# A three-stage kernel: routed rows loaded in blocks and turned by VectorE instead of TensorE, register reads split, a table built inside a branch

## What is computed

```python
x = attention(q, k, v).transpose(0, 2, 1, 3).reshape(3072, 512)
logits = x @ w_gate                      # 8 experts
expert_idx = argmax(logits, axis=1)
for e in range(8):
    mask = expert_idx == e
    out[mask] = gate_w[mask, None] * (np.maximum(x[mask] @ w1[e], 0) @ w2[e])   # 512 -> 1024 -> 512
h = out @ w_in                           # 512 -> 2048
g = (a0 + a1*h + a2*h**2 + a3*h**3) / (1 + |b0|*|h| + |b1|*h**2 + 1e-6)
return g @ w_out                         # 2048 -> 512
```

## Time and profile before

| what | value |
|---|---|
| median of three runs | 1125.18 us |
| the profiled execution | 1128.27 us, its span 1126.7 us |
| mean granted TensorE clock | 0.993 |
| TensorE busy | 1095.6 us, 97% |
| VectorE busy | 898.5 us, 80% |
| ScalarE / GpSimd busy | 593.5 / 259.6 us |
| attention | 0 to about 212 us |
| hand-over to the experts | 212 to 241 us |
| expert tiles | 241 to 585 us |
| dense stage | 585 to 1127 us |

### The profile page before, as it was taken

The page is one execution under the profiler, slowest core; times in us unless marked ns, Lnnn a source line. Parts: engine busy times, 40 slices in busy tenths (PEclk is TensorE's granted clock), DMA queues, the critical chain, the costliest instruction groups (busy, mean ns, idle before and its releaser), DMA issues.

```text
span 1126.7 us, 19523 instructions
## 1 busy us (share of the span) xinstructions
PE 1095.6 (97%) x6023; PEld 891.4 (79%) x6024; DVE 898.5 (80%) x1813; ACT 593.5 (53%) x1060; POOL 259.6 (23%) x191
## 2 busy tenths in 40 slices
PE   6999999799999999999999999999999999999997
PEld 4777777578888888888887888888888888888885
DVE  6778888658788887878769988987986986996975
ACT  6878788322323232322338656655665655655663
POOL 1022111364656566563500001001001001000101
PEclk9999999999999999999999999999999999999999
DMA  8999871296767877875621010010001001000000
GB/s 195 242 281 266 194 200 40 89 327 197 271 220 259 289 240 251 291 242 193 248 94 49 1 39 38 1 38 37 0 1 74 0 0 66 9 0 10 29 1 38
DMA packets 142362, 142.52 MB, mean 126 GB/s; under 512 B 104672, under 2 KB 104672, under 8 KB 141280
## 3 DMA queue, kind: packets, MB, share of 16 engines
q0 software_dynamic: 27584, 92.48, 23.6%
q1 hardware_dynamic: 114720, 49.31, 16.3%
HBM read 118.70 MB, written 23.32 MB: 126 GB/s over the span
## 4 chain that ended last, share of the span: by engine, by line
PE 88%; DVE 8%; ACT 1%; issue 1%; DMA 1%; POOL 0%; SPq 0%; POOLq 0%; ACTq 0%; DVEq 0%
PE bank L1145 23%; PE bank L1147 23%; PE bank L1146 23%; PE bank L990 4%; PE bank L966 4%; PE bank L953 4%; PE bank L931 2%; PE bank L1140 1%; PE bank L1006 1%; DVE poly L1749 1%; DVE poly L1747 1%; PE bank L1215 1%; DVE poly L1762 1%; PE bank L1015 1%; DVE bank L1635 1%
## 5 line engine op out<-in xcount | busy, mean ns | idle before, releaser
L1635 DVE STREAM_TRANSPOSE bank<-hbuf 32x256 f32<-32x256 f32 x464 | 211.5, 456 | 62.0 <-ACT hbuf L766 55.5
L488 POOL TENSOR_TENSOR w_lo<-stage,w_hi 128x2048 fp32r<-128x2048 f32 x32 | 147.6, 4613 | 60.1 <-DMA w_hi<-in_moe_w_dram 28.9
L1145 PE MATMUL bank<-w_hi,gh 128*128 128x512 f32 x384 | 150.5, 392 | 0.3 <-DVE gl L1771 0.3
L1145 PE MATMUL bank<-x2Th,w_hi 128*128 128x512 f32 x384 | 149.5, 389 | 0.5 <-DVE poly L1749 0.5
L1147 PE MATMUL bank<-w_hi,gl 128*128 128x512 f32 x384 | 149.5, 389 | 0.0
L1146 PE MATMUL bank<-w_lo,gh 128*128 128x512 f32 x384 | 149.4, 389 | 0.0
L1147 PE MATMUL bank<-x2Th,w_lo 128*128 128x512 f32 x384 | 149.4, 389 | 0.0
L1146 PE MATMUL bank<-x2Tl,w_hi 128*128 128x512 f32 x384 | 149.4, 389 | 0.0
L623 POOL DMA_INDIRECT out_dram<-stage,ids x24 | 29.6, 1235 | 510.1 <-ACT stage L875 494.4
L1145 PE MATMUL bank<-w_hi,xTh 128*128 (+1 forms) x248 | 97.9, 395 | 2.2 <-DVE xTl L1623 1.5
L1147 PE MATMUL bank<-w_hi,xTl 128*128 (+1 forms) x248 | 97.6, 393 | 0.0
(11 more groups left out here) (221 smaller groups left out, 2221.1 us busy)
## 6 DMA issues: line engine op xcount, KB each, us to landing
w_hi<-in_moe_w_dram POOLq DMA_DIRECT2D x32, 1024.0 KB, 7.6
stage<-in_moe_w_dram POOLq DMA_DIRECT2D x32, 1024.0 KB, 8.0
xg<-routed_x SPq DMA_DIRECT2D x31, 256.0 KB, 4.8
routed_y<-ybuf SPq DMA_DIRECT2D x31, 256.0 KB, 2.7
x<-routed_y SPq DMA_DIRECT2D x6, 1056.0 KB, 5.1
kraw<-in_k_dram SPq DMA_DIRECT2D x24, 256.0 KB
qraw<-in_q_dram SPq DMA_DIRECT2D x24, 256.0 KB
vraw<-in_v_dram SPq DMA_DIRECT2D x24, 256.0 KB, 4.8
```

Source lines behind the costliest of these rows:

```text
L488: pool.tensor_tensor(w_lo[:, at:at + CH], stage[:, c % 2, :], w_hi[:, at:at + CH].bitcast(F32), ALU.subtract).then_inc(chunk_ready, 1)
L1145: pe.matmul(dst, lhs_hi, rhs_hi, start=first, stop=False)
L1635: ins = dve.transpose(HB_ps[k][r * QD:(r + 1) * QD, :, q % 2 * QD:(q % 2 + 1) * QD], rows)
```

## The change

Rows are written to `routed_x` with their columns in another order: `turn_x` writes each transpose in four quarters, so that a row holds its 512 values as [4][4][32]; `normalise`, `normalise_last`, `invert` and `weigh_logits` follow that order, with the reciprocals kept twice. A tile is then loaded by four DMAs of 32 partitions each (512-byte pieces), and one VectorE operation of 128x512, made of 32x32 blocks, gives what TensorE's four transposes gave. VectorE does it (`turn_rows`) ahead of `turn_h` of the tile before; its loop now holds two tiles. The first x tile's four DMAs are issued two by SyncE and two by ScalarE. TensorE reads two registers ahead of `moe_down` and two ahead of `moe_up`. The whole table is built inside each side of the `If`, all 26 linked steps ahead of the first tile; the second tile is turned right behind the first, into a bank and buffers of its own, so TensorE's first tiles run as up(0), first half of up(1), turn of h(0), second half of up(1). The unread products are spread: 7 while the last pair is picked, 16 behind the count, one for each of the steps 16 to 26, four when x(0) is turned. GpSimd's first fetch waits for both first tiles.

```diff
             def load_x(t, r, first=False):
...
-                sp.dma_start(xg[:, r, :], xs[ds(row, P), 0:DM]).then_inc(xg_in[r], 16)
+                load_rows(r, row)
+            def load_rows(r, row, parts=range(4)):
+                for a in parts:
+                    sp.dma_start(xg[a * QD:(a + 1) * QD, r, :].rearrange("n (b c) -> n b c", b=4),
+                                 xs[ds(row, P), a * P:(a + 1) * P].rearrange("(b n) c -> n b c", b=4)).then_inc(xg_in[r], 16)
...
-            sp.dma_start(xg[:, 0, :], xs[0:P, 0:DM]).then_inc(xg_in[0], 16)
+            load_rows(0, 0, (0, 1))
...
-            pool.wait_ge(xg_in[0], 16)
+            pool.wait_ge(xg_in[0], 64)
+            pool.wait_ge(xg_in[1], 64)
...
-            moe_x(0)
-            moe_h(0); moe_x(1); end_ht(0, hTh)
+            for p in range(QT // 2):
+                act.wait_ge(routed[p], 32 * B)
+            for a in (2, 3):
+                act.dma_start(xg[a * QD:(a + 1) * QD, 0, :].rearrange("n (b c) -> n b c", b=4),
+                              xs[0:P, a * P:(a + 1) * P].rearrange("(b n) c -> n b c", b=4)).then_inc(xg_in[0], 16)
+            moe_x(0); moe_x(1, XS_ps, xSh)
+            moe_h(0); end_ht(0, hTh)
...
             def turn_x(b, i, full=False, n=None):
...
-                    mm = pe.transpose(dst[:, j * P:(j + 1) * P], oT[:, i % 2, j, :], ident[:, :])
+                    mm = pe.transpose(quarters(dst[:, :], j), oT[:, i % 2, j, :], ident[:, :])
...
+            def idle_while_picking():
+                pe.wait_ge(chunk_ready, 1)
+                pe.wait_ge(lg_read, LAST + 1)
+                idle_products(1)
+                pe.wait_ge(lg_sum, LAST + 1)
+                idle_products(1)
+                for step in range(4):
+                    pe.wait_ge(lg_step, 4 * (LAST // 2) + step + 1)
+                    idle_products(1)
+                pe.wait_ge(oh_step, LAST // 2 + 1)
+                idle_products(1)
...
-                idle_products(WARM[0])
+                idle_products(WARM)
...
-            idle_products(WARM[1])
+            pe.wait_ge(chunk_ready, 1)
+            for step in range(16, TAB_STEPS + 1):
+                pe.wait_ge(tab_step, step)
+                idle_products(1)
...
-            def pe_tile(t, r, n):
-                off_down, e_down, off_up, e = weights_at(t - 1), expert_of(t - 1), weights_at(t + 1), expert_of(t + 1)
-                moe_turn_x(r, n)
+            def pe_tile(t):
+                off_down, e_down = weights_at(t - 1), expert_of(t - 1)
                 moe_down(t - 1, off_down, e_down)
+                off_up, e = weights_at(t + 1), expert_of(t + 1)
                 moe_up(t + 1, off_up, e)
...
-            moe_turn_x(0, 1)
-            moe_up(0, 0, 0)
+            pe.wait_ge(xg_ps, 1)
+            idle_products(4)
+            moe_up(0, 0, 0, halves=(0,))
             pe.wait_ge(tab_ready, 1)
             off, e = weights_at(1), expert_of(1)
-            moe_turn_x(1, 1)
+            moe_up(0, 0, 0, halves=(1,))
+            moe_up(1, off, e, xSh, xSl, (0,))
             turn_end_h(0)
-            moe_up(1, off, e)
-            pe_tile(1, 0, 2)
+            moe_up(1, off, e, xSh, xSl, (1,))
+            pe_tile(1)
...
-                dve.reciprocal(rcp[:, i % 2, 1, :], rcp[:, i % 2, 0, :]).then_inc(rc_step, 1)
+                dve.reciprocal(rcp[:, i % 2, :, :, :],
+                               den[:, i % 2, :].rearrange("p (j u o) -> p u o j", u=2, o=1).broadcast_to([P, 2, 2, KB]))\
...
+            def turn_rows(t, r, n, dst=X_ps):
+                dve.wait_ge(xg_in[r], 64 * n)
+                if dst is X_ps and not (isinstance(t, int) and t == 0):
+                    dve.wait_ge(xg_lo, t)
+                dve.transpose(dst[:, :].rearrange("p (j b n) -> p j b n", j=KB, b=4),
+                              xg[:, r, :].rearrange("p (b j n) -> p j b n", j=KB, b=4)).then_inc(xg_ps, 1)
...
             with dve.If(banded(dve) > 0):
                 dve_steps()
+                expert_tables()
...
-            def dve_tile(t):
-                turn_h(t, 0); moe_x(t + 1); turn_h(t, 1); moe_ht(t)
-            moe_x(1); end_ht(0, hTh, hTl)
-            with dve.Fori(1, MT - 2) as t:
-                dve_tile(t)
+            def dve_tile(t, r, n):
+                turn_rows(t + 1, r, n); turn_h(t, 0); moe_x(t + 1); turn_h(t, 1); moe_ht(t)
+            end_ht(0, hTh, hTl)
+            with dve.Fori(0, (MT - 3) // 2) as tp:
+                for r in range(2):
+                    dve_tile(2 * tp + r + 1, r, tp + 2)
+            turn_rows(MT - 1, 0, MT // 2 + 1)
```

More of the change, by code:

```diff
@@ L41 @@
 TI = 13
-WARM = (18, 8)
+WARM = 16
+TAB_STEPS = 26
 FAR = -8e9
@@ L139, in build_program @@
         sums = over("sums", [P, 2, H])
-        rcp = over("rcp", [P, 2, 2, H])
+        den = over("den", [P, 2, H])
+        rcp = over("rcp", [P, 2, 2, 2, KB])
         zeros = over("zeros", [P, RW])
@@ L163, in build_program @@
         early = free[1]
+        x2_at = free[1]
         x2 = over("x2", [P, G, RW])
+        xSh, x2_at = place("xSh", [P, KB, P], F32R, x2_at)
+        xSl, _ = place("xSl", [P, KB, P], F32R, x2_at)
         x2Th = over("x2Th", [P, KB, G * P], F32R)
@@ L194, in build_program @@
         HT_ps = bank[2:4]
+        XS_ps = bank[6]
         HB_ps = [bank[2 + k].rearrange("p (j n) -> p j n", j=FB) for k in range(2)]
@@ L694, in evac_logits, with head_cols @@
                 act.activation(lgT[:, :], X_ps[:, 0:P], ACT.Copy).then_inc(lt_sb, 1)
+            def head_cols(row, h):
+                return row.rearrange("p (u v j n) -> p u v j n", u=2, v=2, j=KB)[:, h % 2, :, h // 2, :]
             def normalise_last():
@@ L992, in weigh, with quarters @@
                 mm.then_inc(pv_done, 1)
+            def quarters(row, j):
+                return row.rearrange("p (a j n) -> p a j n", a=4, j=KB)[:, :, j, :]
             def turn_x(b, i, full=False, n=None):
@@ L1032, in route_rank, with idle_products @@
                     .then_inc(rank_ps, 1)
+            def idle_products(times):
+                for n in range(times):
+                    pe.matmul(HT_ps[1][:, :], w_hi[:, 0:P], w_hi[:, 0:512], start=True, stop=True)
+            def idle_while_picking():
[9 more added lines that the diff above has]
+                idle_products(1)
             def pe_steps():
@@ L1108, in count @@
                 pe.matmul(X_ps[:, 0:E], ones[:, :], taken[:, NT // 2 % 2, 0, :], start=True, stop=True).then_inc(count_ps, 1)
[L1110 to L1114, removed]
             with pe.If(banded(pe) > 0):
@@ L1134, in expert_of @@
                 return pe.value_load(exp_i[0:1, 0, ds(t, 1)], min_val=0, max_val=E - 1)
[L1136 to L1141, removed]
             def three(dst, lhs_hi, lhs_lo, rhs_hi, rhs_lo, first, last):
@@ L1147, in three, with moe_up @@
                 return pe.matmul(dst, lhs_lo, rhs_hi, start=False, stop=last)
-            def moe_up(t, off, e):
+            def moe_up(t, off, e, hi=xTh, lo=xTl, halves=(0, 1)):
                 pe.wait_ge(chunk_ready, e * 4 + 2)
                 pe.wait_ge(xg_lo, t + 1)
-                for n in range(2):
+                for n in halves:
                     if not isinstance(t, int) or t > 0:
@@ L1586, in _ @@
                         low_part(b, n)
[L1588 to L1612, removed]
@@ L1613, in _ @@
-            for k in range(2):
-                tl(dve.tensor_tensor(prod[:, k, :, :], past, per_expert(wide[:, 0, k, :]), ALU.mult))
-            tl(dve.tensor_reduce(ttab[:, 0:2, :], prod[:, 0:2, :, :], AX.X, ALU.add))
-            tl(dve.tensor_tensor(ttab[:, 0, :], ttab[:, 0, :], row_no[:, :], ALU.add))
-            tl(dve.scalar_tensor_tensor(out=ttab[:, 2, :], in0=ttab[:, 1, :], scalar=last_at[:, 0:1], in1=ttab[:, 0, :],
-                                        op0=ALU.add, op1=ALU.min))
@@ L1619, in _ @@
-            dve.tensor_copy(row_i[:, :], ttab[:, 2, :]).then_inc(row_ready, 1)
-            def moe_x(t):
-                dve.wait_ge(xg_hi, t + 1)
-                dve.tensor_tensor(xTl[:, :, :], X_ps[:, :].rearrange("p (j n) -> p j n", j=KB), xTh[:, :, :].bitcast(F32),
-                                  ALU.subtract).then_inc(xg_lo, 1)
+                expert_tables()
             def turn_h(t, k):
```

93 lines of the change are left out of this document (64 added, 29 removed).

## The result

The median is 1116.42 us (four runs, 1114.92 to 1118.07); the kernel before took 1125.6 on the same chip (1124.7 to 1126.33). The ratio is 0.9917 with an interval of [0.9904, 0.993]: 9.2 us gained where 15.1 were predicted. The sign is right, but the time lies 0.9 us above the range. The profiled execution took 1118.07 us, span 1116.4, against a span of 1126.7 before: 10.3 us less.

A forecast was written before the change was run, and what follows sets the result against it. TensorE, busy 97% of the span, was taken to bound the kernel. Transposes 11.9, hand-over order 1.8 and clock 1.4 sum to 15.1 us off the median of 1125.18: 1110.1 us, range 1106.1 to 1115.5.

The forecast's parts named there:

- 1. Transposes leave TensorE: Expert tiles: without x transposes on TensorE, 27 tiles give back 0.44 us each, 11.9 us; bounds 2.2 us either way.
- 2. VectorE's new operation: VectorE's gap before turning h: the block transpose takes 0.72 us, fits in 1.34 us idle, and costs nothing.
- The last tile: End of the expert tiles: TensorE waits there for VectorE's scaling, so what this tile saves is waited away.
- 3. Loading in four parts: Loads of x tiles: four DMAs instead of one cost nothing; the longest landing, at most 15.4 us, still fits.
- 4. Reads in two places: TensorE's register reads, two ahead of down and two ahead of up: cost nothing; bounds 0 and 0.2 us a tile.
- 5. The tables: Hand-over: tables inside the `If` start near 212.4, end about 221.2; up(0) stays at 224.66, bounds -0.3 and +0.9 us.
- 6. The order in the hand-over: up(0) to down(0) shrinks from 16.46 to 11.8 us at full clock; counted 1.8 plus 1.4, the middle of 0 to 2.85.
- (c): TensorE exposes waits the transposes covered, at reads or for `hTl`: 0.2 us a tile, 5.4 less gain, 1115.5 us; 9%.
- (a): VectorE sets the pace because the block transpose runs by quadrants, 3.66 us: slower, about 1175 us; 3%.
- (b): The back edge of VectorE's two-tile loop stalls 2.91 us each two tiles: slower, 1133 us; 3%.
- (d): Hand-over: the tables aren't earlier, as the 2.91 us idle aren't the jump: gain 11.8, 1113.4 us; 9%.
- (e): Whole kernel: no difference, some hold-up takes all of the gain; 2%.

The follow-up runs named there:

- e7: Changed kernel, but VectorE turns each tile's rows twice, the second time into a bank nobody reads: 1113.42 us, ratio 0.9915 to the kernel before.
- e1: Changed kernel, but the next tile's `xTl` is made after four of the first eight block transposes of h: 1110.69 us, ratio 0.986 to the kernel before.
- e3: Changed kernel, but VectorE turns the last x tile behind `gate_shift(0)` instead of ahead of it: 1115.13 us, ratio 0.9904 to the kernel before.
- e6: Changed kernel, but SyncE issues all four DMAs of the first x tile, ScalarE none: 1115.17 us, ratio 0.9894 to the kernel before.
- e2: Changed kernel, but TensorE's four register reads of a tile stand together ahead of down: 1122.23 us, ratio 0.9966 to the kernel before.
- e4: Changed kernel, but tables and the first two tiles' turns stand once behind the `If`: 1118.1 us, ratio 0.9922 to the kernel before.
- e0: Changed kernel measured again without any edit: 1115.48 us, ratio 0.9907 to the kernel before.

## Why the prediction was wrong, point by point

**1. Transposes leave TensorE: the mechanism right, the gain not all there.** 11.9 us were predicted, 8.8 - 1.2 = 7.6 came. With `xTl` early the 28 tiles give 319.12 - 304.64 = 14.5 us, more than 28 x 0.44 = 12.3. The pace without transposes is 0.2267 us a product and not the 0.2278 that I read out of the earlier trace rows, so 10.88 a tile and not 10.93: the sets disturbed later products too, which stood in the prediction as a bound of +2.2. Another 0.6 us are two tiles of 11.72 and 11.65 in the trace of before, where the others take 11.37 or 11.38.

**2. VectorE's new operation: the price right, its cover wrong. This is the step that failed.** 0.72 was predicted, 0.727 measured. I looked for its cover in the gap ahead of the h turn, found 1.34 us, and then looked at only one result behind it, `hTl` (0.5 in hand). I put the cost of this step at nothing. But the new operation is not what took the time: e7 doubles it and loses nothing. The lost time is of the other result in the same chain: ReLU of the second half, eight block transposes, `xTl`, up. That chain hangs on the *previous up*, so it doesn't move when down starts sooner; up does, by the 0.44 that the transposes took. Of the 0.64 in hand 0.16 were left, and TensorE starts its product 0.23 behind the end of `xTl` (so in 28 tiles of after, the last among them, and 0.20 behind in the first). With the late second product that is 0.18 us a tile, and 0.20 was lost (11.08 for 10.88). What the change saved it took from a slack that I had not read. Undoing the lateness alone (e1) brings 5.7 us back in the 28 tiles, more than the 3.5 that were missing there.

The Trainium skill ("VectorE: DVE Perf Modes", Rules for kernel authors), which would have left the transposes on TensorE, agrees with the durations here (0.727 us on VectorE; the four transposes cost a tile of TensorE's 11.37 - 10.88 = 0.49). It doesn't fit this kernel, where TensorE sets the pace and VectorE has idle time.

**The last tile** was to lose what it saved (0.4 by the table above) and lost 1.2. The scaling was named, but not that `turn_rows(30)` was put ahead of `gate_shift(0)`, with ScalarE's exp and ReLU behind it. e3 gives 0.7 of it back.

**3. Loading in four parts: right.** In the loop nothing waits for it (VectorE waits 2.2 us for x(0) and x(1), in the hand-over); the longest landing, 11.6 us, lies within the bound of 15.4. In e6 ScalarE's part doesn't show.

**4. Reads in two places: the number right, the reason wrong.** "Nothing" holds for two and two (e1). But the four reads in one place showed no gap before, with transposes behind them, and without these they cost 6.7 us (e2). That the transposes hid them is the likely reading; no run has them back with the reads as they are. Without the split more than half of the gain would be gone (3.8 of 10.5 us left), and I had priced it as a side matter.

**5. The tables: right.** 212.78 for "near 212.4", ready at 221.56 for 221.2, and e4 shows the jump. Where the jump now falls VectorE has 7.06 us to wait for ScalarE's `hTh` in any case (229.11 to 236.17). up(0) at 225.46 instead of 224.66 (bounds -0.3 and +0.9) goes with the first load, which the scatter let go at 220.29 instead of 219.31.

**6. The order in the hand-over: right in its order, the clock open.** At full clock (e0) up(0) to down(0) takes 236.03 - 224.16 = 11.87 us; 11.8 was predicted. In after, with the clock at half for its first products, it is 13.07. So the end of the term with all 2.85 kept occurs, and the end with nothing doesn't: in after 1.2 us are lost, not 2.85. Of the thirteen traces of the changed kernel and its variants ten show 11.9 us and three 13.0 to 13.1. The middle value was low, and luck had a part in it. What decides between the two is open.

**The rivals.** *(c)* was near in price (0.2 us a tile, 1115.5) but named the reads and `hTl`; it was `xTl`. At 9% I held it too unlikely, for the one slack I had read spoke against it. It also set the high end of the range, 1115.5, with every other term at its middle, which left no room for the 0.8 us more that the last tile lost. *(a)* and *(b)* fall: VectorE has 0.73 us idle a tile, and no back edge of its loop shows (its tiles take 11.07 to 11.10 us by turns). *(d)* and *(e)* fall with e4 and the median.

**The sum again**: 7.6 + 2.6 + 0.1 = 10.3 us of span. The gain of the medians is 9.2, since the profiled execution before was 2.7 us above its median and that of after 1.65.

## What to carry to other kernels

When work is taken off the engine that sets the pace, list every result that this engine waits for in the shortened stretch, each with its time in hand, and compare each with what is taken away; the smallest one, not the busiest engine's gap, says how much of the gain arrives. Where one is short, look first for an order on the helping engine that makes the needed result earlier: here one moved call was worth 4.8 us. And an operation that stood between two things (here transposes behind four register reads) may have been hiding the first of them; this was not tested with the transposes back in.

## What the runs showed of the hardware that I had not expected

- Two 128x512 block transposes back to back start 0.63 to 0.64 us apart, though the first is shown as 0.73 long.
- Four register reads beside a loop's back edge, with a product right behind them, delayed TensorE by 0.3 to 1.1 us in every second tile (0.51 to 1.36 us between products instead of 0.23); two and two showed nothing.
- A wait of some 0.1 us for a semaphore doesn't appear under its releaser. The view of waits of after puts all of TensorE's weight loads ahead of up down to "issue":

```profile
PEld bank L1177 <- issue: 11.7, 31, 1.2
```

  With `xTl` early (e1) that row all but goes:

```profile
PEld bank L1177 <- issue: 1.2, 2, 0.7
```

  Only where the wait grew to 0.8 us, at the last tile, was `xTl` named. Its sign in the others was the constant distance, 0.23 us, between the end of `xTl` and the product.
- The way out of an `If` over its other side cost VectorE 2.91 and 2.82 us.
